# Attention with pooled queries before two expert layers: transposing probability tiles by row halves, in one phase with keys, queries and leftovers

## The reference

```
attention:  q, k, v: 4 x 8 heads x 1152 x 64, float32
  q_pool = mean of neighbouring query rows            (576 queries)
  scores = q_pool @ k^T / 8
  attn   = exp(scores - rowmax); attn /= sum + 1e-9
  out    = attn @ v                                   (4 x 576 x 512)
second:     2304 tokens, 512 -> 1024 -> 512, softmax gate, normalisation
third:      2304 tokens sent to one of 8 experts, 512 -> 1024 -> 512
```

## Time and profile before

| | us |
|---|---|
| median of 3 runs | 1127.43 (1125.4 to 1127.88) |
| profiled execution | 1129.12 |
| its span, first to last instruction | 1127.4 |
| mean granted TensorE clock | 0.981 |
| TensorE busy | 1088.0 (97%) |
| VectorE busy | 750.0 (67%) |
| ScalarE busy | 612.9 (54%) |
| GpSimd busy | 381.5 (34%) |
| end of the attention's last copy | 553.5 |

### The profile page before, as it was taken

How to read it: one execution, slowest core, us unless ns; L and a number is a source line. 1 busy time by engine, 2 the same in 40 slices (tenths; PEclk the granted TensorE clock), 3 DMA queues, 4 the chain that set the end, 5 groups by cost and what they waited for, 6 DMA issues and landing times.

```text
span 1127.4 us, 20403 instructions
## 1 busy us (share of the span) xinstructions
PE 1088.0 (97%) x6647; PEld 767.4 (68%) x6647; DVE 750.0 (67%) x1632; ACT 612.9 (54%) x1327; POOL 381.5 (34%) x454
## 2 busy tenths in 40 slices
PE   7899999999999999999899999997989999999996
PEld 4565665556656565655588888886768888888885
DVE  4777787777778777777548999898775633333110
ACT  5676666667666666665465434435356534343221
POOL 4545544454554445445322211215112211111101
PEclk8899999999999999999899999999999999999998
DMA  4221122212112221102520000004556653311100
GB/s 129 64 60 36 53 64 64 62 47 56 44 48 65 64 64 46 40 21 77 150 85 19 28 20 19 28 30 185 171 180 239 228 182 113 106 38 49 39 21 1
DMA packets 92705, 85.59 MB, mean 76 GB/s; under 512 B 49006, under 2 KB 69486, under 8 KB 92464
## 3 DMA queue, kind: packets, MB, share of 16 engines
q1 hardware_dynamic: 88592, 72.92, 21.0%
q0 software_dynamic: 4000, 11.28, 3.1%
HBM read 74.73 MB, written 11.27 MB: 76 GB/s over the span
## 4 chain that ended last, share of the span: by engine, by line
PE 44%; DVE 2%; issue 2%; POOL 1%; ACT 1%; DMA 1%; DVEq 0%; ACTq 0%; POOLq 0%
PE h_ps L694 8%; PE h_ps L696 8%; PE h_ps L695 8%; PE o_ps L694 5%; PE o_ps L696 5%; PE o_ps L695 5%; PE t_ps L1170 2%; PE t_ps L1062 1%; PE h_ps L1137 1%; PE h_ps L1186 1%; DVE junk L1266 1%; DMA w_raw_e<-in_moe_w 1%; DVE w_split L1480 0%; POOL x_lo L973 0%; PE h_ps L1084 0%
## 5 line engine op out<-in xcount | busy, mean ns | idle before, releaser
L346 POOL TENSOR_SCALAR probs<-probs,scales 128x576 f32<-128x576 f32 x288 | 209.8, 748 | 263.6 <-DVE scales L547 263.6
L642 ACT ACTIVATE probs<-s_ps,lows 128x576 f32<-128x576 f32 x288 | 211.0, 737 | 146.5 <-DVE lows L518 146.1
L518 DVE TENSOR_REDUCE lows<-s_ps 128x1 f32<-128x576 f32 x288 | 205.2, 753 | 59.1 <-PE s_ps L423 51.3
L371 PEld LDWEIGHTS t_ps<-ident,probs 128*128 128x128 f32 x1152 | 123.8, 141 | 108.4 <-issue 100.4
L423 PE MATMUL s_ps<-kt,qt 64*128 64x288 f32 x1024 | 163.9, 438 | 4.8 <-ACT probs L642 4.8
L371 PE MATMUL t_ps<-ident,probs 128*128 128x128 f32 x1152 | 158.8, 281 | 2.8 <-POOL probs L346 2.0
L472 PE MATMUL pv_ps<-pt,values 128*64 128x512 f32 x576 | 155.2, 618 | 1.0 <-DVE x_t L582 1.0
L556 DVE COPY pt<-t_ps 128x512 f32<-128x512 f32 x144 | 99.4, 690 | 43.7 <-PE t_ps L371 43.6
L423 PEld LDWEIGHTS s_ps<-kt,qt 64*128 64x128 f32 x1024 | 89.3, 190 | 43.4 <-issue 24.5
L992 POOL DMA_INDIRECT out<-junk,target_rows x25 | 29.5, 1182 | 261.0 <-ACT junk L1699 260.7
L637 ACT COPY pt<-t_ps 128x512 f32<-128x512 f32 x144 | 84.4, 586 | 28.5 <-PE t_ps L371 24.5
(11 more groups left out here) (257 smaller groups left out, 2056.2 us busy)
## 6 DMA issues: line engine op xcount, KB each, us to landing
w_raw_e<-in_moe_w SPq DMA_DIRECT2D x60, 512.0 KB, 5.5
k_raw<-in_k SPq DMA_DIRECT2D x32, 256.0 KB, 2.8
q_raw<-in_q SPq DMA_DIRECT2D x32, 256.0 KB, 3.2
token_rows<-x_rows SPq DMA_DIRECT2D x18, 256.0 KB, 2.0
values<-in_v SPq DMA_DIRECT2D x32, 128.0 KB, 2.7
values<-in_v SPq DMA_DIRECT2D x64, 64.0 KB, 2.7
w_raw<-in_moe_w_in SPq DMA_DIRECT2D x4, 512.0 KB, 5.0
w_raw<-in_moe_w_out SPq DMA_DIRECT2D x4, 512.0 KB, 3.8
```

The costliest lines, as they stand in the source:

```text
L346: nc.gpsimd.tensor_scalar(where, where, scales[:, g % 2, s, c:c + 1], 1.0, ALU.mult, ALU.mult).then_inc(norm_done if c else half_scaled, 1)
L371: last = nc.tensor.transpose(bank[:, i * P:(i + 1) * P], source, ident[:])
L518: nc.vector.tensor_reduce(lows[:, g % 2, s, c:c + 1], s_ps[c][:, :, 0:part], AX.XY, ALU.max, negate=True).then_inc(low_done[c], 1)
L642: nc.scalar.activation(two_halves(probs[g % 2][:, s, :])[:, :, columns(c)], s_ps[c][:, :, 0:part], ACT.Exp, bias=lows[:, g % 2, s, c:c + 1 ...
```

## The change

- The eight full tiles and the blocks of the visit are transposed in one phase (`turn_phase`), each as two halves of 64 rows: the low half into `t_ps[0]`, the high half into `t_ps[1]`. Low halves and high halves of different tiles are issued in turn, so that two neighbours never write the same bank. The high halves of the visit's blocks wait for its low halves (`low_thirds`).
- TensorE's order in a slot is scores, transposes, product. Transposes are due one slot later (lag 11 for 10), the product with them. The probabilities lie in a ring of 19 tiles.
- Queries of both heads are summed by one GpSimd instruction and transposed in one visit (Q); VectorE scales them into `qx`, and four DMAs of SyncE move them into `qt`. Visits for the next pair are in slots 0, 1, 2, 7; left-overs in 4, 5, 6.
- VectorE copies keys and queries, ScalarE the left-overs. In a slot both do the scores' work first, then the copies.
- The weighted sums and totals are computed on GpSimd; VectorE adds 1e-9 and takes the reciprocal; GpSimd multiplies with `raises` and the reciprocal in one instruction.
- TensorE gets extra transposes of the identity in the first pair, at the end of the attention and at the start of the second stage. The high parts of `w_in` are made by VectorE in the last pair, GpSimd's low parts wait for `t_done`. The first low part of x is made by VectorE.

```diff
-    kq_slots = {0: KA, 1: QA, 2: TAILS, 6: KB, 7: QB}
-    rest_slots = (3, 4, 5)
+    kq_slots = {0: KA, 1: Q, 2: TAILS, 7: KB}
+    first_kq_slots = {4: KA, 5: Q, 6: TAILS, 7: KB}
+    rest_slots = (4, 5, 6)
+    lag = slots + 2
+    ring = 2 * slots + 1
...
+            def move_queries(n):
+                sp.wait_ge(kq_out, kq_count(n, Q))
+                for h in range(2):
+                    first = h * (full + 1)
+                    for u in range(2):
+                        sp.dma_start(qt[n % 2][rows(u), first:first + full, :].rearrange("p t n -> p (t n)"),
+                                     qx[rows(h), :]).then_inc(q_moved, 16)
...
             def normalise(g, b):
-                pool.wait_ge(scales_ready, len(batches) * g + b + 1)
-                for s in range(*batches[b]):
+                par, (first, end) = g % 2, batches[b]
+                steps = 2 * (len(batches) * g + b)
+                pool.wait_ge(raises_done, len(batches) * g + b + 1)
+                pool.sem_inc(passed, 1)
+                nc.gpsimd.tensor_tensor(weighted[:, par, first:end, :], raises[:, par, first:end, :],
+                                        sums[:, par, first:end, :], ALU.mult).then_inc(total_steps, 1)
+                pool.wait_ge(total_steps, steps + 1)
+                pool.sem_inc(passed, 1)
+                nc.gpsimd.tensor_tensor(total[:, par, first:end], weighted[:, par, first:end, 0],
+                                        weighted[:, par, first:end, 1], ALU.add).then_inc(total_steps, 1)
+                pool.wait_ge(recips_done, len(batches) * g + b + 1)
+                for s in range(first, end):
                     for c in range(2):
...
             for g in range(pairs):
-                if g + 1 < pairs:
-                    add_queries(g + 1, 1)
                 normalise(g, 0)
+                normalise(g, 1)
                 if g + 2 < pairs:
-                    add_queries(g + 2, 0)
+                    add_queries(g + 2)
                     add_tail(g + 2)
-                for b in range(1, len(batches)):
-                    normalise(g, b)
+                normalise(g, 2)
+                normalise(g, 3)
+            pool.wait_ge(t_done[1], key_tiles * (pairs - 1))
...
+            def turn_half(out, source, u):
+
+                return nc.tensor.transpose(out, source[rows(u), :], ident[rows(u), rows(u)])
+
+            def turn_phase(i, thirds, third_done):
+
+                pair, j = i // key_tiles, i % key_tiles
+                if j == 0:
+                    pe.wait_ge(norm_done, slots * (pair + 1))
+                if i > 0:
+                    pe.wait_ge(t_out[0], i)
+                    pe.wait_ge(t_out[1], i)
+                tiles = [probs(pair, s)[:, j * P:(j + 1) * P] for s in range(slots) if s != full]
+
+                def tile_half(n, u):
+                    return turn_half(t_ps[u][:, n * dim:(n + 1) * dim], tiles[n], u)
+
+                def third_half(n, u):
+                    return turn_half(third_ps[:, n * P + u * dim:n * P + (u + 1) * dim], thirds[n], u)
+
+                count = len(thirds)
+                for n in range(len(tiles) + count):
+                    if n < count:
+                        low_third = third_half(n, 0)
+                        if n == count - 1:
+                            low_third.then_inc(low_thirds, 1)
+                            low_third_count[0] += 1
+                    else:
+                        low_half = tile_half(n - count, 0)
+                    if n < len(tiles):
+                        high_half = tile_half(n, 1)
+                        if n == len(tiles) - 1:
+                            high_half.then_inc(t_done[1], 1)
+                    else:
+                        if n == len(tiles):
+                            pe.wait_ge(low_thirds, low_third_count[0])
+                        high_third = third_half(n - len(tiles), 1)
+                if thirds:
+                    high_third.then_inc(third_done, 1)
+                low_half.then_inc(t_done[0], 1)
...
                 for h in range(2):
                     last = nc.tensor.matmul(pv_ps[rows(h), :], values[pair % 2][:, h, j, :],
-                                            pt[i % 2][:, h * main:(h + 1) * main], start=(j == 0),
+                                            pt[i % 2][:, :, h * main // 2:(h + 1) * main // 2], start=(j == 0),
                                             stop=(j == key_tiles - 1))
...
                     i, m = turned_index(at, s), multiplied_index(at, s)
-                    if i is not None:
-                        turn_tiles(i, 0)
-                        turn_tiles(i, 1)
-                    third_visit(at, s, at)
                     if at < pairs:
                         score_tile(at, s, at)
+                    thirds, third_done = third_blocks(at, s, at)
+                    if i is not None:
+                        turn_phase(i, thirds, third_done)
+                    elif thirds:
+                        turn_blocks(third_ps, thirds, third_done)
+                    if at == 0:
+                        warm(pv_ps, 4 if s < 2 or has_kq(at, s) else 8)
                     if m is not None:
                         multiply(m)
...
+            warm(s_ps[0][:, 0, :], 8)
...
+            def invert_totals(g, b):
                 par, (first, end) = g % 2, batches[b]
+                dve.wait_ge(total_steps, 2 * (len(batches) * g + b) + 2)
+                nc.vector.tensor_scalar(total[:, par, first:end], total[:, par, first:end], 1e-9, None,
+                                        ALU.add).then_inc(guarded, 1)
+                dve.wait_ge(guarded, len(batches) * g + b + 1)
+                nc.vector.reciprocal(recips[:, par, first:end], total[:, par, first:end]).then_inc(recips_done, 1)
...
                     if at < pairs:
                         lowest(at, s, 0)
                         lowest(at, s, 1)
                         for b, (first, end) in enumerate(batches):
                             if s == end - 1:
                                 merge_lows(at, b)
-                            if s == end and b < 2:
-                                merge_scales(at, b)
+                            if s == end:
+                                invert_totals(at, b)
+                    if s == 0 and 1 <= at <= pairs:
+                        invert_totals(at - 1, len(batches) - 1)
+                    if i is not None:
+                        copy_turned(i)
+                    if has_kq(at, s):
+                        next_kq(at, s)
...
+                    if at == pairs - 1 and s in high_slots:
+                        c = high_slots.index(s)
+                        dve.wait_ge(w_loaded[c], 16)
+                        nc.vector.tensor_copy(w_hi[:, c, :], w_raw[:, c, :]).then_inc(w_in_hi_done, 1)
...
                     if at < pairs:
                         exponentials(at, s, 0)
+                        if s == 1 and at >= 2:
+                            act.wait_ge(t_done[1], key_tiles * (at - 1))
                         exponentials(at, s, 1)
...
+                    if i is not None:
+                        copy_turned(i)
+                    if has_rest(at, s):
+                        copy_rest(at, s)
...
-            split_x(0)
...
+            for i in range(12):
+                nc.tensor.transpose(o_ps[:, 0:P], ident[:], ident[:])
...
+            dve.wait_ge(x_hi_done, 1)
+            nc.vector.tensor_tensor(x_lo[:, 0, :].rearrange("p (b n) -> p b n", n=P), columns_of(x_t, 0),
+                                    x_hi[:, 0, :].rearrange("p (b n) -> p b n", n=P).bitcast(F32),
+                                    ALU.subtract).then_inc(first_x_lo, 1)
```

More of the change, by code:

```diff
@@ L96, in build_attention @@
         k_tail = in_arena("k_tail", [P, 2, dim])
-        q_raw = [in_arena(f"q_raw{h}", [P, full, 2 * dim]) for h in range(2)]
+        q_raw = in_arena("q_raw", [P, full, 2, 2 * dim])
         q_tail = in_arena("q_tail", [P, 2 * dim])
-        q_sum = [in_arena(f"q_sum{h}", [P, full, 2, dim]) for h in range(2)]
+        q_sum = in_arena("q_sum", [P, full, 2, dim])
+        first_q_sum = in_arena("first_q_sum", [P, full, 2, dim])
+        kt_size = 2 * half
         kt = [in_arena(f"kt{i}", [P, 2, half]) for i in range(2)]
         qt = [in_arena(f"qt{i}", [P, slots, P]) for i in range(2)]
-        probs = [in_arena(f"probs{i}", [P, slots, seq]) for i in range(2)]
+        placed = [(slots + 2 + i) % ring for i in range(ring)]
+        tiles_by = {i: in_arena(f"probs{i}", [P, seq]) for i in placed[:-1]}
         assert 2 * w_chunks * d_ff <= at_column[0] - arena - slots * seq
+        assert all(slots * (pairs - 1) + s not in range(0) and (slots * (pairs - 1) + s) % ring in placed[slots + 1:]
+                   for s in range(slots))
+        assert in_chunks * d_ff <= 2 * (pieces * dim + main * 2) + 2 * P + kt_size
         w_raw = in_arena("w_raw", [P, stages, d_ff])
```

(41 more changed lines are left out.)

240 lines of the change are left out of this document (109 added, 131 removed).

## The result

The changed kernel takes 1081.54 us (1080.06 to 1082.67, 4 runs), the kernel before beside it 1127.46; the ratio is 0.9595 [0.9576, 0.9614]. The forecast was 1084. The profiled execution took 1082.6 us, with a span of 1080.7.

The account below looks back on a forecast made before the run. TensorE bounds the attention now, VectorE next. Steady pairs -33, second pair -4, first pair -3, attention's end +1, first layer's start -3.8: total -43 us, from 1129.1 to 1086 profiled, 1084 as median; range 1057 to 1108.

Parts of the forecast that it names:

- Halves beside each other: Attention transposes on TensorE: two row halves run beside each other, 0.058 us a pair of halves; a whole transpose takes 0.11.
- Rivals A: Transposes: the load or queueing keeps a pair of halves at 0.11 us; 31.7 us a pair of heads, 1107; chance 0.13.
- B: Transposes: half loads of both row groups run one after another, 0.22 us a pair of halves; 1252; chance 0.04.
- VectorE sets the pace: Steady attention pairs: VectorE's 26.5 us of work exceeds TensorE's 26.2, plus 1.9 waiting for GpSimd's totals and 1.8 for scores.
- Rival C: Totals: GpSimd's additions take 0.1 and precede the query sums, so VectorE's 1.9 wait goes; 28.3 a pair, 1056; chance 0.2.
- Rival D: Totals: VectorE's and GpSimd's small instructions hold each other up, 0.8 us more per batch; 33.5 a pair, 1132; chance 0.06.
- A steady pair of 30.2 us: Attention, 13 steady pairs of heads: each takes 30.2 us in place of 32.75, together -33 us.
- The second pair: Attention's second pair of heads: 30.7 us by the walk, 34.8 before, -4 us.
- The first pair: Attention's first pair: transposes in idle time keep TensorE's clock up, 24.5 us for 27.4, -3 us.
- The order of the slot: Attention slots on TensorE: scores, transposes, then product, so the gap between scores and transposes goes; 2.88 us a four-block slot.
- The end: Attention's end: GpSimd's later low parts of weights hold back second weights' loads; 58.2 us from last pair's start, 57.5 before, +1.
- The start of the second stage: First layer's start: low part on VectorE ends 1.3 us sooner, added transposes save 2.5 us of slow clock, -3.8 us.

Follow-up runs that it names:

- first experiment: Changed kernel, but each phase issues all its low halves first and then all its high halves: 1108.96 us, ratio 0.9836.
- fourth experiment: Changed kernel with the weighted sums and totals computed on VectorE again, GpSimd only scaling: 1060.02 us, ratio 0.9402.
- ninth experiment: Changed kernel with totals on VectorE and the third pair's queries loaded before the first values, in the first round only: 1056.5 us, ratio 0.9368.
- seventh experiment: Changed kernel, but GpSimd scales by `raises` alone, the division by the totals left out: 1079.57 us, ratio 0.9578.
- third experiment: Changed kernel without the added transposes of the identity in its three places: 1084.78 us, ratio 0.9628.

## Why the prediction was right or wrong

- **Halves beside each other, 0.058 us a pair: right.** 0.057 by the phases' means; twelve pairs in 0.87 us where 0.7 to 0.8 was forecast (the last half is followed by the product only after 0.15), with two records of one start. The first experiment shows that the turn of the halves does it. There was luck in the size: the row that it was taken from, the leftovers' product, alternates between halves of the columns (`128*64` in its shape) and not of the rows. By the Trainium skill ("TensorE: Matmul & The Clock Gate", LDWEIGHTS) a load costs its 128 columns whatever its rows, which by its formula makes an estimate of 107 ns a half. The trace disagrees: halves of one row group, each with a load of its own, start 0.063 us apart in the first experiment. Rivals A (31.7 a pair) and B (41.4) fall with it; the records of the half loads, 139 ns, are no pace.
- **VectorE sets the pace, with 1.9 us a pair of waiting for totals: right.** Measured 2.0, in slots 8 and 0 of VectorE's order as forecast, but 0.49 and 1.6 us where 0.85 and 1.06 were walked, by instructions of 0.2 us behind the query sums and the scaling. Rival C had 28.3 a pair without this wait; taking it away gave 28.28, though C built it from 26.5 us of VectorE's work, which measures less (below), so that the close match is luck. Rival D's dear hand-overs don't show from one addition to the next (0.18 us), but what it read from the 690 ns row does: the merge of four columns takes 0.77 us in the changed kernel. That costs nothing there, and 0.6 us a pair in the fourth and the ninth experiment.
- **A steady pair of 30.2 us: 0.5 too much, 6.7 us over 13 pairs.** Several sizes were off, in opposite directions. Copies were taken at the 0.69 of their records, but they follow each other sooner. The timeline of VectorE:

```profile
256.22 0.69 DVE L651 COPY pt<-t_ps 128x512 f32<-128x512 f32 x1
256.82 0.28 DVE L635 TENSOR_SCALAR kt<-third_ps 128x128 f32<-128x128 f32 x1
```

  A copy costs 0.60: for thirteen copies of 512 columns in a pair 1.2 us less, and VectorE is busy 24.4 us a pair where I had 26.5; the sign that I had set, 26 to 27 of 30, was not met. Against it, VectorE waits 2.7 us for scores where I had 1.8, as TensorE is busy for 27.7 us and not 26.2, and GpSimd's scaling with two factors takes 829 ns and not the 748 of one, 1.4 us more of GpSimd for 18 chunks, which by the seventh experiment lengthens the pair by 0.87. VectorE's smaller work was the larger of these. Two slips in the sums change nothing: 18 maxima at 0.71 are 12.8 and not 12.9, and B with half of D makes 0.07 for slower.
- **The second pair, 34.8 to 30.7: wrong in sign**, it went to 37.4; this is the step that failed in its mechanism. The forecast let GpSimd go from batch to batch without a look at the load before the query sum. That load stands behind the values' in SyncE's order, and by the change the wait for it passes on to VectorE, where the totals had been VectorE's own. Both halves of this were tried: the totals back on VectorE alone give 34.9 us, the queries early alone 32.0, and both 27.7 (loads of the first round), 9.7 less, where a steady pair gains 1.1: some 8.6 us were this.
- **The first pair: -4.7 for -3.** Slot 0 lost 1.0 us (3.45 to 2.48) and slots 4 to 8 together 3.8 (16.5 to 12.7), those that ran at the lower clock before. Two blocks of scores in the timeline of the kernel before:

```profile
21.94 2.29 PE L423 MATMUL s_ps<-kt,qt 64*128 64x288 f32 x8 [0.85 <-ACT probs L642]
24.99 2.29 PE L423 MATMUL s_ps<-kt,qt 64*128 64x288 f32 x8 [0.75 <-ACT probs L642]
```

  They took 1.48 in the earlier trace rows. So the clock that stays up gives most of it, as forecast, but not by the added transposes. What kept it up (visits in other slots, the new order, one sum of queries in place of two) was not tried apart.
- **The order of the slot: its gaps are gone (scores 1.08 us of a slot for 1.17), its worth was nothing** (29.67 and 29.70) until the totals left GpSimd, then 1.05 a pair. I had counted it with TensorE's work, which while VectorE waits for totals doesn't set the length of the pair.
- **The end, +1 forecast and -1.9 measured:** wrong in sign too; the low parts of weights would have held back less than the walk gave, but that was not tried by itself, and the cause stays open. **The start of the second stage**, -3.8, was -2.9; the added transposes give 0.9 of it.
- **Idle time of TensorE: there, as forecast, but less.** 2.0 us a pair, where 26.2 of 30.2 would have left 4.0; its busy time is 27.7.

The sum, -43 for -46.7, owes some of its closeness to errors that cancel: it gave the second pair 6.6 us too much and the second stage 0.9, and the steady pairs 6.7 too little and the first pair and the end 4.6.

## What to carry to other kernels

Small operations moved to an idle engine are not free where the busy engine must wait for them: their price is what stands ahead of them in that engine's order, loads included, and what stands behind the wait on the other. Before moving them, ask whether the wait can come after the instructions that free buffers; here the place of the reciprocals alone was worth 9 us, and giving the work back 21. In this kernel a new order of issue on TensorE was worth nothing while VectorE waited for totals, and 1.05 us a pair once it didn't. And before a difference of 0.3 us a pair is put down to an edit, look at the single pairs: with the totals on VectorE, one small instruction that takes 0.16 or 0.77 us beside GpSimd's scaling made most of such a difference.

## What the runs showed of the hardware

- Half transposes (64x128, float32) on two row groups, taken in turn, pass at 0.057 us a pair; halves of one row group at 0.063 each, another bank making no difference. Whole 128x128 transposes pass at 0.109 each (eight last 1.023 and twelve 1.459 us in the kernel before).
- A second per-row factor adds 81 ns to GpSimd's scaling of 128x576 (748 to 829).
- A merge of four columns on VectorE takes 771 ns in the mean beside GpSimd's scaling in the changed kernel; in the fourth experiment it takes 161 to 167 ns in ten steady pairs and 770 or 771 in three. The product of `raises` and sums with two columns took 539 ns in the fourth experiment and 220 with the reciprocals last.
- The clock in the first pair stayed at 1.00 through a stretch with TensorE busy for 2.96 of 5 us (third experiment), and before it fell to 0.60 behind one with 4.04 of 5. Why, the rows don't show.
